# A linear-attention scan and two feed-forward layers on one core: the first layer unrolled, its feed-forward work run as one stream across tiles

## The reference

```python
cur = np.einsum('bhd,bhe->bhde', u[None] * kt, vt)
y[:, :, t] = np.einsum('bhd,bhde->bhe', rt, state + cur)
state = wt[:, :, :, None] * state + np.einsum('bhd,bhe->bhde', kt, vt)
```

## Time and profile before

| | us |
|---|---|
| three timed runs | 1113.47, 1115.38, 1120.17 |
| median | 1115.38 |
| the profiled execution, its own time | 1111.6 |
| its span, first to last instruction | 1109.8 |

### The profile page before, as it was taken

The page is one execution under the profiler, slowest core; times in us unless marked ns, Lnnn a source line. Parts: engine busy times, 40 slices in busy tenths (PEclk is TensorE's granted clock), DMA queues, the critical chain, the costliest instruction groups (busy, mean ns, idle before and its releaser), DMA issues.

```text
span 1109.8 us, 24301 instructions
## 1 busy us (share of the span) xinstructions
PE 1029.2 (93%) x10088; PEld 829.3 (75%) x10088; DVE 613.5 (55%) x938; ACT 494.2 (45%) x835; POOL 114.2 (10%) x74
## 2 busy tenths in 40 slices
PE   3378999799979997999799999999999999999998
PEld 3366787578767875787678888888888888888886
DVE  6998863786468646864776445443334333333332
ACT  1233444244434443444334477655445454454543
POOL 5943100310021002100310000000000000000000
PEclk8579999899999998999999999999999999999999
DMA  7423013102210121011203310101001010010000
GB/s 299 126 80 144 3 73 119 41 2 73 92 68 2 73 102 58 2 73 73 87 2 116 109 63 1 57 1 49 8 1 57 0 57 0 0 57 0 28 0 29
DMA packets 23433, 61.61 MB, mean 56 GB/s; under 512 B 2353, under 2 KB 6833, under 8 KB 22961
## 3 DMA queue, kind: packets, MB, share of 16 engines
q1 hardware_dynamic: 23344, 60.27, 15.3%
HBM read 50.82 MB, written 9.44 MB: 54 GB/s over the span
## 4 chain that ended last, share of the span: by engine, by line
PE 86%; DVE 8%; issue 4%; DMA 1%; ACT 0%; SPq 0%; DVEq 0%; ACTq 0%
PE down_bank L389 37%; PE up_bank L389 26%; PE g_bank L389 17%; PE y_bank L389 4%; DVE att L781 3%; DVE att L779 2%; DVE att L767 1%; DVE att L789 1%; PE y_bank L432 1%; DMA att<-kT_dram 1%; PE g_bank L497 0%; DVE att L759 0%; DVE scratch L876 0%; DVE state L813 0%; SPq L243 0%
## 5 line engine op out<-in xcount | busy, mean ns | idle before, releaser
L389 PE MATMUL down_bank<-g_hi,wout_lo 128*128 128x512 f32 x576 | 236.1, 410 | 0.0
L600 ACT CAST g_hi<-scratch 128x512 fp32r<-128x512 f32 x192 | 119.1, 620 | 255.0 <-DVE scratch L876 137.0
L389 PE MATMUL down_bank<-g_hi,wout_hi 128*128 128x512 f32 x576 | 228.4, 397 | 0.0
L389 PE MATMUL down_bank<-g_lo,wout_hi 128*128 128x512 f32 x576 | 228.4, 396 | 0.0
L389 PE MATMUL up_bank<-x_hi,win_lo 128*128 128x512 f32 x432 | 179.1, 415 | 5.8 <-issue 4.1
L846 DVE TENSOR_TENSOR g_lo<-scratch,g_hi 128x512 fp32r<-128x512 f32 x192 | 135.6, 706 | 87.4 <-ACT g_hi L600 86.1
L389 PE MATMUL up_bank<-x_hi,win_hi 128*128 128x512 f32 x432 | 172.6, 399 | 0.0
L389 PE MATMUL up_bank<-x_lo,win_hi 128*128 128x512 f32 x432 | 172.6, 399 | 0.0
L389 PE MATMUL g_bank<-att 64*64 64x64 f32 x4576 | 112.5, 245 | 50.0 <-DVE att L781 36.1
L389 PEld LDWEIGHTS g_bank<-att 64*64 64x64 f32 x4576 | 99.5, 143 | 77.9 <-issue 77.9
L389 PEld LDWEIGHTS down_bank<-g_hi,wout_lo 128*128 128x128 f32 x576 | 109.3, 190 | 25.9 <-DVE g_lo L846 0.5
(11 more groups left out here) (76 smaller groups left out, 1147.4 us busy)
## 6 DMA issues: line engine op xcount, KB each, us to landing
att<-rT_dram SPq DMA_DIRECT2D x12, 512.0 KB, 3.4
att<-kT_dram SPq DMA_DIRECT2D x12, 512.0 KB, 4.1
att<-wT_dram SPq DMA_DIRECT2D x12, 512.0 KB, 6.0
ynat<-rN_dram SPq DMA_DIRECT2D x12, 384.0 KB, 5.0
k_steps<-kN_dram SPq DMA_DIRECT2D x12, 384.0 KB, 6.5
att<-vN_dram SPq DMA_DIRECT2D x12, 384.0 KB, 6.9
x_dram<-scratch SPq DMA_DIRECT2D x18, 256.0 KB, 4.4
ynat<-x_dram SPq DMA_DIRECT2D x6, 768.0 KB, 4.3
```

Source lines behind the costliest of these rows:

```text
L389: return nc.tensor.matmul(out, lhsT, rhs, start=start, stop=stop, **kw)
L600: return nc.scalar.copy(out, in_)
```

## The change

- **Unrolled.** All loops over tiles become straight code, in both layers and on every engine.
- **One stream.** Feed-forward slots are numbered through (F = 16c + f). `down(F-2)` runs in slot F across a tile's border, so slots 0 and 1 hold the downs of the tile before, and the copies of a finished tile out of PSUM (`tile_out_of_psum`) come on ACT in slot 1 of the next tile, before `down` of its slot 0, which waits for them. x has two buffers (`x[c % 2]`); layer two's x is prepared in slots 8 to 10 of the tile before.
- **Levels.** In tiles c = 1 to 4 each slot holds at most one level: group 0's levels 0 to 2 of the tile after next run in slots 13 to 15, levels 3 to 6 in slots 0 to 3, group 1's in slots 4 to 10. Tile 0 holds group 0's in slots 0 to 6 and group 1's in 4 to 10. Rows are in slots 5, 6, 12, 13 (tile 0: 8, 9, 12, 13), turns of x two slots later.
- **ACT** copies `k_turned` after a slot's three activations, where it did before them.
- **Pair products** read r in another order (the two halves of a chunk one after the other instead of interleaved) and write their PSUM bank through a permuted pattern whose neighbours are 8 bytes apart, so that the bank's layout stays the same.
- **Buffers.** `r_nat` is a buffer of its own and also holds the tiles on their way out; the weight pieces are staged in three scratch buffers and three parts of `ynat`, the last four pieces in the three scratch buffers alone. The mask of the last level is dropped.
- **Loads.** SP's order becomes: stores of the tile before the last, group 0, the natural loads, group 1. At the start the natural loads of tile 1 come ahead of both groups. Layer two's weights come in eight transfers instead of two. POOL's products for tile c+2 follow when its natural loads have landed, in tile c.

```diff
+STAGE = [i % NSTAGE if i < 24 else (i - 24) % 3 for i in range(len(W1_PIECES))]
+ROWS_FIRST, ROWS = (8, 9, 12, 13), (5, 6, 12, 13)
+TURNS_FIRST, TURNS = (10, 11, 14, 15), (7, 8, 14, 15)
+SUMS = ((3, 4), (13, 14), (10, 11))
+        def levels_at(c, f):
+            k, now, late = c + 1, [], []
+            if c == 0:
+                now += [(k, 0, f)] if f < NL else []
+                late += [(k, 1, f - 4)] if 4 <= f < 4 + NL else []
+            elif k < NC:
+                now += [(k, 0, f + 3)] if f < 4 else []
+                now += [(k, 1, f - 4)] if 4 <= f < 4 + NL else []
+            if k + 1 < NC and f >= 13:
+                now.append((k + 1, 0, f - 13))
+            return now, late
...
-            return r.rearrange("p (s n two m) -> p n two m s", s=2, two=2, m=2 ** l)[:, :, 1, :, :]
+            return r.rearrange("p (s n two m) -> p s n two m", s=2, two=2, m=2 ** l)[:, :, :, 1, :]
...
+                            out = product_banks(k, g)[a][hs, j * PAD:(j + 1) * PAD]
+                            if l < NL - 1:
+                                out = out.rearrange("p (n m s) -> p s n m", m=2 ** l, s=2)
...
+            def load_group(k, g):
+                sp.wait_ge(state_ready, k * B - 2 + 2 * g)
...
+            def load_natural(k):
+                if k > 0:
+                    sp.wait_ge(ds_filled, 2 * B if k == 1 else (k - 1) * 2 * B + B)
+                if k > 2:
+                    sp.wait_ge(tile_stored, (k - 2) * 16 * KT)
...
+                if STAGE[i] in STAGE[:i]:
+                    before = max(n for n in range(i) if STAGE[n] == STAGE[i])
+                    sp.wait_ge(w1_hi_ready, before + 1)
+                    sp.wait_ge(w1_lo_ready, before + 1)
...
+            load_natural(1)
+            load_group(1, 0)
+            load_group(1, 1)
+            for c in range(NC - 2):
+                if c > 0:
+                    store_tile(c - 1)
+                load_group(c + 2, 0)
+                load_natural(c + 2)
+                load_group(c + 2, 1)
...
@@ tensor engine, layer one @@
+            for c in range(NC):
                 for f in range(FT):
+                    now, late = levels_at(c, f)
+                    row, turned = row_at(c, f), turned_at(c, f)
                     up(c, f)
+                    if turned is not None:
+                        turn_x(c + 1, turned)
+                    for k, g, l in now:
+                        pair_products(k, g, l)
+                    if row is not None:
+                        turn_k(c + 1, row)
+                    if c * FT + f >= 2:
+                        down(c * FT + f - 2, range(KT - 1))
+                    if row is not None:
+                        attend(c + 1, row)
+                    if c * FT + f >= 2:
+                        down(c * FT + f - 2, range(KT - 1, KT))
+                    for k, g, l in late:
+                        pair_products(k, g, l)
+                    if row is not None:
+                        state_step(c + 1, row)
...
@@ scalar engine @@
+            def layer1_slot(c, f):
...
+                if F:
+                    hi_of_g(F - 1)
+                if turned is not None:
+                    x_hi_of(c + 1, turned)
+                act.wait_ge(up_done, F + 1)
...
+                nc.scalar.activation(act_buf[f % 2], act_buf[f % 2], ACT.Square).then_inc(pre_ready, 1)
+                if row is not None:
+                    k_turned_of(c + 1, row)
+                for k, g, l in now + late:
+                    if l == NL - 1:
+                        last_level(k, g)
...
+                if f == 1 and c > 0:
+                    tile_out_of_psum(c - 1)
...
@@ vector engine @@
+            def layer1_slot(c, f):
...
+                for k, g, l in before:
+                    level(k, g, l)
+                if F:
+                    lo_of_g(F - 1)
+                if turned is not None:
+                    x_lo_of(c + 1, turned)
+                for k, g, l in now:
+                    level(k, g, l)
+                for k, g, l in before:
+                    next_decays(k, g, l)
+                dve.wait_ge(pre_ready, F + 1)
...
+                for k, g, l in now:
+                    next_decays(k, g, l)
+                if row is not None:
+                    output(c + 1, row)
```

More of the change, by code:

```diff
@@ L499, in turn_x @@
                 last.then_inc(xt_filled, 1)
-            def attention(k, f, part, plan=PLAN):
-                level, row = places(f, plan)
-                if part == "early":
-                    if level[0] is not None:
-                        pair_products(k, 0, level[0])
-                    if row is not None:
-                        turn_k(k, row)
-                if part == "middle" and row is not None:
-                    attend(k, row)
-                if part == "late":
-                    if level[1] is not None:
-                        pair_products(k, 1, level[1])
-                    if row is not None:
-                        state_step(k, row)
@@ L571, in _ @@
-            pe.wait_ge(zeroed, 1)
-            for f in range(FT):
-                if f == PLAN_FIRST[2][0]:
-                    pe.wait_ge(consts_in, 32)
-                for part in ("early", "middle", "late"):
-                    attention(0, f, part, PLAN_FIRST)
-                if f - 1 in PLAN_FIRST[2]:
-                    turn_x(0, f - 1 - PLAN_FIRST[2][0])
-            pe.wait_ge(w1_lo_ready, len(W1_PIECES))
-            with pe.Fori(0, NC - 1) as c:
-                layer1_tile(c, True)
@@ L631, in w2_hi_of, with k_turned_of @@
                         copy(hi, raw).then_inc(w2_hi_ready, 1)
+            def k_turned_of(k, b):
+                act.wait_ge(kt_filled, k * B + b + 1)
+                for g in range(2):
+                    act.wait_ge(rk_multiplied[g], min(k + 2 if k > 0 and b >= 2 else k + 1, NC))
+                if k > 0 or b >= 2:
+                    act.wait_ge(ds_filled, k * 2 * B + 2 * b - 2)
+                copy(k_turned[:, (b % 2) * HP * P:(b % 2 + 1) * HP * P], banks(k, b)[0][:, :]).then_inc(kt_copied, 1)
             def last_level(k, g):
@@ L638, in last_level @@
                     copy(later_half, products[0:HALF, :]).then_inc(masked[g], 1)
-            def attention(k, f, part, plan=PLAN):
-                level, row = places(f, plan)
-                if part == "early":
-                    if row is not None:
-                        act.wait_ge(kt_filled, k * B + row + 1)
-                        act.wait_ge(rk_multiplied[1], k + 1)
-                        if later(k) or row >= 2:
-                            act.wait_ge(ds_filled, k * 2 * B + 2 * row - 2)
-                        copy(k_turned[:, (row % 2) * HP * P:(row % 2 + 1) * HP * P],
-                             banks(k, row)[0][:, :]).then_inc(kt_copied, 1)
-                if part == "late" and level[0] == NL - 1:
-                    last_level(k, 0)
-                if part == "early" and f and places(f - 1, plan)[0][1] == NL - 1:
-                    last_level(k, 1)
@@ L928, in level_masks @@
+            dve.wait_ge(w1_lo_ready, len(W1_PIECES))
+            for c in range(NC):
+                for f in range(FT):
+                    layer1_slot(c, f)
+            for c in range(NC, 2 * NC):
+                for f in range(FT):
+                    layer2_slot(c, f)
+            lo_of_g(2 * NC * FT - 1)
 def level_masks():
```

609 lines of the change are left out of this document (282 added, 327 removed).

## The result

| | us |
|---|---|
| the changed kernel, median of 4 runs | 1075.39 (1075.09 to 1077.59) |
| the kernel before, median of 4 runs on the same chip | 1116.62 (1113.47 to 1120.17) |
| ratio, 95% interval | 0.963 (0.960 to 0.967) |
| profiled execution after, its own time / span | 1075.09 / 1073.3 |
| profiled execution before, its own time / span | 1111.6 / 1109.8 |

Two executions of later kernels that took far longer than their others (5466.97 us of the old kernel with the new orders, 1258.17 us of the one with group 0 loaded first) are left out of all numbers here. Forecast were 1093 and a range of 1074 to 1113: the time lies in the range, 18 us under the forecast, where rival (2) had put it (1077).

What follows compares the result with a forecast made beforehand. PE's matmuls, busy for 93% of the span, were taken as the bound; only startup and tiles 0 to 4 could shorten. Terms summed to -20.2 us, 1091.4, and with half of 3.8 us added 1093; range 1074 to 1113.

Steps and rivals of the forecast that it cites:

- rival (2): Pair products: reads held levels at 1.33 and 1.57 us, and all come down to 1.15; 1077 us, chance 0.18.
- H: Patterns of the 60 pair products of levels 0 to 5: taken as 0 us, ends -15.6 and +34.8.
- Rival (1): Pair products: the permuted PSUM writes make levels slower, 1128 us at the worst end; chance 0.23.
- A: Unrolling: the issue gaps in tiles 1 to 4 all go, -12.1 us; ends 0 and -12.1.
- B: Levels one per slot, tiles 1 to 4: 16.9 us of waits for DVE go, POOL collision adds 7.5; net -9.4.
- C: Clock in tiles 1 to 4: two of six half-clock stretches stay, -6.8 us; ends 0 and -10.2.
- D: `k_turned` behind the activations in row slots: `attend` waits 8 x 0.6 us, +4.8; late level 0 in slot 13, +0.9.
- E: Startup: weight piece 27 waits for its buffer and delays row 1's keys, +2.4 us; ends 0 and +3.9.
- F: Tile 1's natural loads ahead of group 0's: tile 0 waits 3.6 us against 4.1, taken as 0; ends -4 and +4.
- G: Layer two: stays PE-bound, with a tile's copies out of PSUM hidden behind `up`; no change.
- (3): Tiles: the POOL collision costs DVE as much as the start did, clock falls as often; 1109 us, chance 0.09.
- (4): Unrolled code: gaps of fetching come back at each burst of loads; 1105 us, chance 0.05.

## Why the forecast was off by 18 us, point by point

**H, the level products, is the step that failed**: "I take 0, nearest to the rows of levels 1 to 5: the new order reads the same places as often." The places are the same, their order is not, and the order is what costs: 0.17 us in each of 40 levels and 0.41 in each of 20, 15.0 us in all. The kernel with the old read alone gives 14.6 in its span, the one with both old orders 19.0 in its time, waits and clock included. The working had both ends and the right best one (-15.6). What it missed stood in its own rows: levels 0 and 1 differ from levels 2 to 5 only in how they read, and cost 1.57 for 1.33. That says that reading sets the price, so a change of the read order could not be taken as nothing. It stood under rival (2) as the argument for it and got 0.18.

**Rival (1) had the larger chance, 0.23, and nothing in a row for it.** No strided write of PE was in the trace, and the write turned out free. The row that argued against it (a level sends 512 columns in 1.0 us, a layer's matmul in 0.23, so a write has four times as long) fits, but no run here writes a layer's matmul through a stride, so whether the time per write is the reason stays open.

**A, the issue gaps: right**, and by its cause: PE's loop unrolled alone takes all seven away. They stood at a tile's first matmul or in the middle of its first level, with DVE idle. The part that the forecast didn't have is that 3.2 us of them had covered DVE's lateness at the tile's start; in the whole change 6.2 us of waits for DVE are left in tiles 1 to 4, all behind POOL, so the new order of levels takes care of that.

**B, waits for DVE: right in mechanism and size.** 7.5 us of collision were forecast, 2.5 in each of tiles 1 to 3; measured were 6.2, 2.06 each. It was in slot 10 alone: the level of slot 8 was through when POOL began (247.52 against 247.89), so the first hit of 0.7 did not come. (The rows give 4.3 us from the end of one level's products to the next, where the working has 4.1; nothing hung on it.)

**C, the clock: right, -6.8 in tiles 1 to 4.** Two stretches are left, each behind a wait of 2.07 us; the third wait of the same length has none behind it. Which ones have is not fixed: it was tiles 1 and 3 here, 1 and 2 in the second trace of the same kernel. Tile 0 has a second stretch (+1.7), which I had not counted. Window of one of them, from the changed kernel:

```profile
258.00:262.00 4.00, 4.00 (x29) 3.30 (x26) 3.41 (x7) 3.32 (x6) 0.00 (x0) 0.58 0.00 0
```

**D, the copy of the keys: right**, 8 waits and 5.0 us for 4.8; seven are 0.51 and one, in tile 0, 1.42: POOL's products start at 162.51 there, DVE's line 879 takes 2.33 us beside them, and ACT's operations ahead of the copy come late. The 0.9 for `output` in slot 13 did not appear, since the level before it is 0.17 shorter too.

**E, the startup: the wait was right, the sum only by luck.** Piece 27 costs what was said and more (3.6 to 4.8 us by the kernel that casts it later, the clock included, 2.4 forecast). But the startup had been 2.9 us faster until then: ACT's copies of the last level began at 60.44 where they began at 63.31. Of that, 1.3 are there from the start: group 1's keys land earlier and its first product starts at 9.97 instead of 11.28. Where the rest comes from was not looked into. I had costed only what the new staging adds.

**F: right** as nothing (-0.9); the wait for group 0's data came, 2.5 us, in place of waits for DVE. **G: right**, layer two is 402 us and has no wait.

**Rivals (3) and (4)** did not happen in the changed kernel. (3) came up when POOL was moved, in another slot and with more half clock, and when group 0's data landed earlier. (4) came up nowhere: from 50 us on, each idle time called "issue" in the traces of straight code (0.4 to 3.4 us) ends 0.1 us after DVE's decays do. Only in the startup, at 16 to 17 us, are there some of 0.4 to 0.8 us with no such end before them.

## What to carry to other kernels

When two groups of matmuls of one shape differ in time and only their read pattern differs, the read pattern is the price, and an edit that reorders the read must be costed by that difference and not at zero. An issue gap can cover another engine's lateness: take it away and that engine shows up. Before an idle time without a named releaser is called a gap of fetching, look whether an engine that PE depends on has just ended something; where the start follows such an end by the same 0.1 us each time, it is a wait. A collision of POOL with DVE moved to another slot is still paid there, unless what DVE feeds in that slot is off the path first. And a stretch at half clock is weighed by its length and by PE's work in it, not by counting stretches.

## What was not expected of the hardware

- Moving data read with neighbouring columns 256 bytes apart made a level of 64 small float32 products 1.33 us (1.57 at levels 0 and 1) instead of 1.16 at full clock. At half clock the same level took 1.99 in either order (28.44 us before, 91.33 us in the kernel with the keys first, granted clock 0.50), so the price of the read is hidden there.
- A write to PSUM in steps of 8 bytes, from 64-column products, took 1.16 us, as a contiguous one.
- Seven issue gaps of 0.7 to 2.8 us (12.1 in all) went with PE's loop, and straight code had none of that size from tile 0 on, under loads at 408 GB/s too. The Trainium skill, "Runtime: NRT & Kernel Launch", section "Instruction fetch mechanics", ties such gaps to taken branches. By that rule, the runs agree: the seven go when the loop is unrolled.
- While POOL's products run, DVE's operations from SBUF to SBUF of 128x512 take 2.3 us for 0.7, one of 128x32 1.86 for 0.23, and its masks out of PSUM are as fast as ever (1.34 for two, with POOL running at 254.44, and 1.35 without at 239.87).
